# Attention and two gated products on one core: at a block border of the second product, VectorE does the border's sums first and the next operand's low halves after them

## The chip, the cores and the metric

The kernel runs on one core of one Trainium2 chip. The metric is the device time of one execution in microseconds (us). Smaller is better. The core's engines work in parallel and meet at semaphores: TensorE (PE in the profile; PEld is its weight load), VectorE (DVE), ScalarE (ACT), GpSimd (POOL) and SyncE (SP), which here only issues DMAs.

## The reference

```python
def _moe_ref(x, w_in, w_out) -> np.ndarray:
    h = x @ w_in
    g = h * np.cos(h)
    return (g @ w_out).astype(np.float32)
def _moe2_ref(x, w1, w2, w3, w_out) -> np.ndarray:
    h = np.maximum(np.maximum(x @ w1, x @ w2), x @ w3)
    return (h @ w_out).astype(np.float32)
def reference(**kwargs):
    ...
    attn_out = _attn_ref(**attn_kwargs)
    x = np.ascontiguousarray(attn_out.transpose(0, 2, 1, 3)).reshape(B * S, H * D)
    x = _moe_ref(x=x, **moe_kwargs)
    return _moe2_ref(x=x, **moe2_kwargs)
```

The attention is a chunked one over 3072 tokens. The first layer has 512 inputs, 2048 hidden features and 512 outputs, the second 512, 768 (three times) and 512. All in float32. The "second product" of this document is `g @ w_out` of the first layer.

## The kernel before

The program runs through stages: attention together with the first product `x @ w_in` and the gate (to about 360 us), the second product (to about 594 us), then the second layer. Every float32 operand of a product is split into a high part (a cast by ScalarE to the type fp32r) and a low part (what is left, a subtraction by VectorE), and each product is three matmuls, high by high, high by low and low by high (`three`, L617 to L619).

The second product is done with the seven products of Winograd's form of a 2 by 2 block multiplication. The tokens stand in six **blocks** of 512 (`NBLK1`, index b). Each block has eight **units** (`FPAIRS`, index i, in all 48 units n = 8 b + i); a unit adds the contribution of 256 hidden features. In a unit TensorE does the products in the order 1, 6, 7, 5, 2, 3, 4 (`ORDER1`), each into a PSUM bank of its own that stays open for all eight units, with six matmuls of 256 columns: 42 matmuls in a unit. In the last unit of a block each product's last matmul raises `whole_done[p]` (for product 4 it is `unit_done`), and in the first unit of the next block a bank is opened again only when its contents have been read (`open_bank`): bank 1 after `y1_copied`, 6 after `u2_done`, 7 after `u3_done`, 5 after `y5_copied`, 2 after `y11_done`, 3 after `y12_done`, 4 after `y21_done`. This place is a **block border**. The borders stand at units 7, 15, 23, 31, 39 and 47; here they are called border 0 to border 5. "Border 0" is thus the end of unit 7 and the start of unit 8.

The operand g of a unit is made by a pipeline. SyncE loads it from DRAM into one of two raw buffers (`load_g`, L365), VectorE makes its sums (`sums_g(n)`: four instructions of 256 columns, L1191 to L1197), ScalarE the high part in two pieces (`high_g`, L914) and VectorE the low part in two pieces (`low_g(n, 0)` and `low_g(n, 1)`, L1207, 1024 and 768 columns), the second of which raises `g_ready`. TensorE starts unit n only with `g_ready` at n + 1. Three operand slots take turns. The raw buffer is free when the low part is made: `load_g(n + 2)` waits for `g_ready` of n, so a load follows the low halves of the unit two before it.

VectorE's list is written out by hand. In turn n it makes the sums and low halves of unit n + 2, two units ahead of TensorE. At a border it also makes the border's sums: `u2` (L1334, waits for `whole_done[6]`), `u3` (L1337, `whole_done[7]`), `y11` (L1343, `whole_done[2]`), two sums in `y12` (L1345 and L1348, the second after `whole_done[3]`), `y22` (L1350) and `y21` (L1353, after `unit_done`). SyncE stores the four results one turn later (`store_y`, L374): its list there is `load_g(n + 4)` for border unit n, the stores of the border, then the next load.

Of the kernel before, what the change touches and what calls it, by code (L numbers as in the profile page):

```python
# [36 lines left out]
FPAIRS = NF // 2  # L37
# [5 lines left out]
UNITS1 = NBLK1 * FPAIRS  # L43
# [35 lines left out]
def program(nc, qk_in, v_in, w1_in, w2_in, y_dram, out):  # L79
    ctx = ExitStack()  # L80
    with ctx:
# [43 lines left out]
        def operand(i):  # L125
            return slot(i).rearrange("p (h q c) -> p h q c", h=2, q=7)
# [183 lines left out]
        def y_total(b):  # L310
            return 16 * sum(Y_PIECES[b % 2:b + 1:2])
# [796 lines left out]
        def _(dve):  # L1108
# [75 lines left out]
            def low_w1(p):  # L1184
                dve.wait_ge(w1_high, p + 1)
                w = operand(p)
                dve.scalar_tensor_tensor(out=w[:, 1, :, :], in0=raw_w1(p), scalar=-2 * PI, in1=w[:, 0, :, :].bitcast(F32),
                                         op0=ALU.mult, op1=ALU.subtract).then_inc(w1_ready, 1)
# [10 lines left out]
            def sums_g(n):  # L1199
                dve.wait_ge(g_landed[n % 2], 16 * (n // 2) + 16)  # L1200
                sums_cols(graw[n % 2], g_sums, 4 * n)

            def low_g(n, part):
                dve.wait_ge(g_high, 2 * n + part + 1)
                q = slice(0, 4) if part == 0 else slice(4, 7)
                g = operand(9 + n % 3)
                low = dve.tensor_tensor(g[:, 1, q, :], graw[n % 2][:, q, :], g[:, 0, q, :].bitcast(F32), ALU.subtract)  # L1207
                if part:
                    low.then_inc(g_ready, 1)

            def low_w2(u):
                dve.wait_ge(w2_high, u + 1)
                w = operand(SLOT_A[u])
                raw = raw_d[W2_RING[u]]
                dve.tensor_tensor(w[:, 1, :, :], raw, w[:, 0, :, :].bitcast(F32), ALU.subtract).then_inc(w2_ready, 1)

            def y_sum(blk, i):
                dve.wait_ge(y_landed, 32 * blk + 32)
                if i:
                    dve.wait_ge(y_sums, 4 * blk + i)  # L1220
                b11, b12, b21, b22, e = [raw_y[:, q, :, :] for q in range(5)]
                if i == 2:
                    dve.wait_ge(y_ready, 7 * blk + 2)
                if i == 3:
                    dve.wait_ge(y_ready, 7 * blk + 4)
                o, in0, in1 = ((e, b12, b11), (b12, b22, b12), (e, b22, e), (e, b21, e))[i]
                dve.tensor_tensor(o, in0, in1, ALU.subtract).then_inc(y_sums, 1)  # L1227

            def y_low(blk, p):
                dve.wait_ge(y_high, 7 * blk + YORDER.index(p) + 1)  # L1230
                y = y_slot(p)
                dve.tensor_tensor(y[:, 1, :, :], source_y(p), y[:, 0, :, :].bitcast(F32), ALU.subtract).then_inc(y_ready, 1)  # L1232
# [27 lines left out]
            for t in range(NBLK):  # L1260
                n = NSUB * (t + 1)
                last = t == NBLK - 1
                for f in range(NF):
# [11 lines left out]
                    if f % 2:  # L1275
                        i = FPAIRS * t + f // 2
# [44 lines left out]
            for n in range(UNITS1):  # L1321
                b, i = divmod(n, FPAIRS)
                if n == 0:
                    low_w1(6)
                elif n == 3:
                    low_w1(7)
                if n and n + 2 < UNITS1:
                    sums_g(n + 2)
                if i == FPAIRS - 1:
                    dve.wait_ge(whole_done[6], b + 1)  # L1330
                    dve.wait_ge(y1_copied, b + 1)
                    if b:
                        dve.wait_ge(y_stored[(b - 1) % 2], y_total(b - 1))
                    dve.tensor_tensor(y12, y11, ps[:, BANK1[6], :], ALU.add).then_inc(u2_done, 1)  # L1334
                    dve.wait_ge(whole_done[7], b + 1)
                    dve.wait_ge(u2_done, b + 1)
                    dve.tensor_tensor(y21, y12, ps[:, BANK1[7], :], ALU.add).then_inc(u3_done, 1)  # L1337
                if n and n + 2 < UNITS1:
                    low_g(n + 2, 0)
                    low_g(n + 2, 1)  # L1340
                if i == FPAIRS - 1:
                    dve.wait_ge(whole_done[2], b + 1)
                    dve.tensor_tensor(y11, y11, ps[:, BANK1[2], :], ALU.add).then_inc(y11_done, 1)  # L1343
                    dve.wait_ge(y5_copied, b + 1)
                    dve.tensor_tensor(y12, y12, p5_kept, ALU.add).then_inc(u25_done, 1)  # L1345
                    dve.wait_ge(whole_done[3], b + 1)
                    dve.wait_ge(u25_done, b + 1)
                    dve.tensor_tensor(y12, y12, ps[:, BANK1[3], :], ALU.add).then_inc(y12_done, 1)  # L1348
                    dve.wait_ge(u3_done, b + 1)
                    dve.tensor_tensor(y22, y21, p5_kept, ALU.add).then_inc(y22_done, 1)  # L1350
                    dve.wait_ge(unit_done, FPAIRS * (b + 1))
                    dve.wait_ge(y22_done, b + 1)
                    dve.tensor_tensor(y21, y21, ps[:, BANK1[4], :], ALU.add).then_inc(y21_done, 1)  # L1353
                if n == 17:
                    low_w2(0)
                if n in (30, 31):
                    y_sum(0, n - 30)
                elif n == 41:
                    y_low(0, 1)
                    y_low(0, 5)  # L1360
                elif n == 42:
                    y_sum(0, 2)
                    y_low(0, 2)
                    y_low(0, 6)
                elif n == 43:
                    y_sum(0, 3)
                    y_low(0, 3)
                    y_low(0, 7)
                elif n == 44:
                    y_low(0, 4)  # L1370
                elif n == 45:
                    low_w2(1)
                elif n == 47:
                    low_w2(2)
# [140 lines left out]
```

## Time and profile before

| | us |
|---|---|
| median of 3 runs | 953.59 |
| lowest and highest of them | 952.93, 955.41 |
| the profiled execution, its own time | 953.36 |
| its span, first to last instruction | 951.6 |
| TensorE busy in the span | 935.8 |
| VectorE busy | 681.8 |
| ScalarE busy | 512.8 |
| GpSimd busy | 183.5 |

The span is what the trace covers; 1.8 us lie around it. Busy times of engines overlap, so their sum is not the span. A start time in a row counts from the span's beginning.

### The profile page before, as it was taken

The numbers are of one execution on the slowest core, as the hardware profiler recorded it, in microseconds if no ns is written. First come the engines' busy times: TensorE is split into PE (matmuls) and PEld (weight loads), VectorE is DVE, ScalarE is ACT, GpSimd is POOL, SyncE is SP. The second block draws the span as 40 slices with busy tenths as digits, with TensorE's granted clock in tenths as the row PEclk, the third lists the DMA queues.
The fourth block names the chain that finished last, engine by engine and source line by source line (L and its number), as shares of the span: only waits on it lengthen the run. The fifth ranks groups of instructions, "written<-read, shape, count | busy, mean of one in ns | idle before, by whom it ended". The sixth has DMA issues, their size and how long they took to land.

```text
span 951.6 us, 21413 instructions
## 1 busy us (share of the span) xinstructions
PE 935.8 (98%) x9100; PEld 918.7 (97%) x9100; DVE 681.8 (72%) x938; ACT 512.8 (54%) x689; POOL 183.5 (19%) x207
## 2 busy tenths in 40 slices
PE   6999999999999999999999999999999999999998
PEld 5889999999999999999999999999999999999998
DVE  5767667676766789989988889767446347678771
ACT  3879697877868884434343345434224224444441
POOL 0011112121211212001100003931000002657720
PEclk8999999999999999999999999999999999999999
DMA  8953456454653443434364342331130201325522
GB/s 299 372 190 131 141 180 211 152 189 156 207 184 129 134 167 122 156 124 150 121 208 136 127 134 92 130 123 56 54 113 34 100 34 56 122 100 201 191 97 78
DMA packets 55422, 135.60 MB, mean 142 GB/s; under 512 B 5152, under 2 KB 14368, under 8 KB 55328
## 3 DMA queue, kind: packets, MB, share of 16 engines
q1 hardware_dynamic: 44960, 98.58, 30.6%
q0 software_dynamic: 10368, 35.66, 10.2%
q8 instruction: 72, 1.18, 0.5%
q14 instruction: 22, 0.18, 0.1%
HBM read 87.03 MB, written 47.19 MB: 141 GB/s over the span
## 4 chain that ended last, share of the span: by engine, by line
PE 80%; DVE 9%; ACT 5%; DMA 3%; issue 2%; SPq 0%; POOL 0%; DVEq 0%; ACTq 0%
PE ps L617 25%; PE ps L618 25%; PE ps L619 25%; DVE units L1207 3%; PE ps L658 2%; PE ps L631 2%; PE ps L669 1%; ACT units L914 1%; PE ps L644 1%; DMA out<-work 1%; DMA early_qk<-qk_in 1%; DVE units L1232 1%; DMA work<-w_in 1%; ACT work L894 1%; ACT work L889 1%
## 5 line engine op out<-in xcount | busy, mean ns | idle before, releaser
L617 PE MATMUL ps<-units 128*128 128x384 f32 (+1 forms) x1940 | 606.6, 313 | 4.3 <-DVE units L1159 1.4
L619 PE MATMUL ps<-units 128*128 128x384 f32 (+1 forms) x1940 | 601.3, 310 | 0.0
L618 PE MATMUL ps<-units 128*128 128x384 f32 (+1 forms) x1940 | 601.1, 310 | 0.0
L617 PEld LDWEIGHTS ps<-units 128*128 128x128 f32 x1940 | 368.0, 190 | 8.2 <-DVE units L1112 1.7
L618 PEld LDWEIGHTS ps<-units 128*128 128x128 f32 x1940 | 368.2, 190 | 0.0
L619 PEld LDWEIGHTS ps<-units 128*128 128x128 f32 x1940 | 368.0, 190 | 0.0
L914 ACT CAST units<-work 128x1024 fp32r<-128x1024 f32 x96 | 85.8, 939 | 119.6 <-DVE work L1193 107.2
L1063 ACT COPY work<-ps 128x384 f32<-128x384 f32 (+1 forms) x144 | 63.5, 454 | 147.4 <-PE ps L619 146.2
L1207 DVE TENSOR_TENSOR units<-work,units 128x1024 fp32r<-128x1024 f32 x96 | 102.1, 1104 | 9.4 <-ACT units L914 9.4
L514 POOL DMA_DIRECT2D g_dram<-work x64 | 46.7, 729 | 299.4 <-DVE work L1170 299.4
L1170 DVE SCALAR_TENSOR_TENSOR work<-work 128x768 f32<-128x768 f32 x64 | 61.2, 957 | 36.4 <-ACT work L896 36.4
L1165 DVE SCALAR_TENSOR_TENSOR work<-work 128x768 f32<-128x768 f32 x64 | 60.7, 949 | 35.2 <-ACT work L889 35.2
L886 ACT ACTIVATE work<-ps 128x768 f32<-128x768 f32 x64 | 51.7, 807 | 53.2 <-PE ps L619 53.2
L1386 DVE TENSOR_TENSOR work<-work,ps 128x384 f32<-128x384 f32 (+1 forms) x48 | 24.8, 517 | 57.3 <-PE ps L619 57.0
L889 ACT ACTIVATE work<-ps,rounder 128x768 f32<-128x768 f32 x64 | 57.3, 896 | 1.9 <-DVE work L1170 1.9
L896 ACT ACTIVATE work<-work 128x768 f32<-128x768 f32 x64 | 54.2, 846 | 2.0
L894 ACT ACTIVATE work<-work 128x768 f32<-128x768 f32 x64 | 54.6, 853 | 0.2
L538 POOL DMA_DIRECT2D work<-w_in x18 | 9.8, 547 | 221.2 <-DVE units L1232 130.5
L1242 DVE TENSOR_TENSOR units<-work,units 128x1792 fp32r<-128x1792 f32 x18 | 41.2, 2289 | 15.3 <-ACT units L954 15.3
L1407 DVE TENSOR_TENSOR work<-work,ps 128x384 f32<-128x384 f32 (+1 forms) x48 | 24.9, 518 | 26.4 <-PE ps L619 26.0
L1412 DVE TENSOR_TENSOR work<-work 128x1152 f32<-128x1152 f32 x24 | 34.8, 1452 | 0.8
L939 ACT CAST units<-work 128x768 fp32r<-128x768 f32 x28 | 22.9, 836 | 22.8 <-DVE work L1227 18.7
(88 smaller groups left out, 771.1 us busy)
## 6 DMA issues: line engine op xcount, KB each, us to landing
g_dram<-work POOLq DMA_DIRECT2D x64, 384.0 KB, 3.5
work<-g_dram SPq DMA_DIRECT2D x48, 512.0 KB, 3.8
work<-qk_in SPq DMA_DIRECT2D x18, 768.0 KB, 6.1
work<-w_in POOLq DMA_DIRECT2D x40, 256.0 KB, 3.6
h_dram<-work SPq DMA_DIRECT2D x24, 384.0 KB, 3.0
work<-h_dram SPq DMA_DIRECT2D x18, 512.0 KB, 4.4
work<-y_dram SPq DMA_DIRECT2D x8, 768.0 KB, 5.9
out<-work SPq DMA_DIRECT2D x24, 256.0 KB, 2.5
```

The source lines that it names most:

```text
L617: pe.matmul(o, wh, mh, start=start, stop=False, skip_group_check=onto)
L618: pe.matmul(o, wh, ml, start=False, stop=False, skip_group_check=onto)
L619: return pe.matmul(o, wl, mh, start=False, stop=stop, skip_group_check=onto)
L886: act.activation(hid(i), hidden_banks(i), ACT.Copy, scale=1.0 / (2 * PI)).then_inc(u_copied, 1)
L889: act.activation(ang(i), hidden_banks(i), ACT.Identity, scale=1.0 / (2 * PI), bias=rounder[:, :])\
L894: act.activation(ang(i), ang(i), ACT.Sin, scale=BELOW_PI).then_inc(sin_done, 1)
L896: act.activation(ang(i), ang(i), ACT.Square, scale=ROOT_TWO).then_inc(square_done, 1)
L914: act.copy(operand(9 + n % 3)[:, 0, q, :], graw[n % 2][:, q, :]).then_inc(g_high, 1)
L1063: act.copy(tile[:, 0:span_of(n)], bank).then_inc(copied, 1)
L1165: dve.scalar_tensor_tensor(out=ang(i), in0=ang(i), scalar=ROUND, in1=hid(i), op0=ALU.subtract, op1=ALU.subtract).then_inc(r_done, 1)
L1170: dve.scalar_tensor_tensor(out=hid(i), in0=ang(i), scalar=1.0, in1=hid(i), op0=ALU.subtract, op1=ALU.mult).then_inc(g_done, 1)
L1207: low = dve.tensor_tensor(g[:, 1, q, :], graw[n % 2][:, q, :], g[:, 0, q, :].bitcast(F32), ALU.subtract)
```

## The change

In the turn of a border unit, except the last border (unit 47, which has no unit n + 2), the two `low_g(n + 2, ...)` move from between `u3` and `y11` to behind `y21`. All else stays: the same instructions, waits and increments.

```diff
@@ -1335,7 +1335,7 @@
                     dve.wait_ge(u2_done, b + 1)
                     dve.tensor_tensor(y21, y12, ps[:, BANK1[7], :], ALU.add).then_inc(u3_done, 1)
-                if n and n + 2 < UNITS1:
+                if n and n + 2 < UNITS1 and not (i == FPAIRS - 1 and n + 2 < UNITS1):
                     low_g(n + 2, 0)
                     low_g(n + 2, 1)
                 if i == FPAIRS - 1:
@@ -1351,6 +1351,9 @@
                     dve.wait_ge(y22_done, b + 1)
                     dve.tensor_tensor(y21, y21, ps[:, BANK1[4], :], ALU.add).then_inc(y21_done, 1)
+                if i == FPAIRS - 1 and n + 2 < UNITS1:
+                    low_g(n + 2, 0)
+                    low_g(n + 2, 1)
                 if n == 17:
                     low_w2(0)
```

VectorE's list at border 0 before the change (L1334 is `u2`, L1337 `u3`, L1207 the two pieces of the low part, L1343 to L1353 the other sums, L1191 the first sum of the next operand):

```order
360 L1334 TENSOR_TENSOR work<-work,ps 128x512
361 L1337 TENSOR_TENSOR work<-work,ps 128x512
362 L1207 TENSOR_TENSOR units<-work,units 128x1024
363 L1207 TENSOR_TENSOR units<-work,units 128x768
364 L1343 TENSOR_TENSOR work<-work,ps 128x512
365 L1345 TENSOR_TENSOR work<-work 128x512
366 L1348 TENSOR_TENSOR work<-work,ps 128x512
367 L1350 TENSOR_TENSOR work<-work 128x512
368 L1353 TENSOR_TENSOR work<-work,ps 128x512
369 L1191 TENSOR_TENSOR work<-work 128x256
```

And with the change, at the same place:

```order
360 L1334 TENSOR_TENSOR work<-work,ps 128x512
361 L1337 TENSOR_TENSOR work<-work,ps 128x512
362 L1343 TENSOR_TENSOR work<-work,ps 128x512
363 L1345 TENSOR_TENSOR work<-work 128x512
364 L1348 TENSOR_TENSOR work<-work,ps 128x512
365 L1350 TENSOR_TENSOR work<-work 128x512
366 L1353 TENSOR_TENSOR work<-work,ps 128x512
367 L1207 TENSOR_TENSOR units<-work,units 128x1024
368 L1207 TENSOR_TENSOR units<-work,units 128x768
369 L1191 TENSOR_TENSOR work<-work 128x256
```

Five sums stand ahead of the two pieces that followed `u3`. Borders 1, 2 and 4 read the same; at border 3 one more instruction (L1227) follows the block in both. The lists of the other engines are unchanged. This is SyncE's before and after, from the loads ahead of border 0 to those behind border 1 (L365 loads an operand g, L374 stores a border's results):

```order
45 L365 DMA work<-g_dram 128x2x512 x11
46 L374 DMA y_dram<-work 128x2x256
47 L374 DMA y_dram<-work 128x2x128 x4
48 L374 DMA y_dram<-work 128x2x256
49 L365 DMA work<-g_dram 128x2x512 x8
50 L374 DMA y_dram<-work 128x2x256 x4
```

The last load of row 45 is the one of unit 11. It waits for the low part that has moved, and the stores of border 0 stand behind it in the same list.

## Rows read from the trace of the kernel before

**Rows 1.** The page, part 1: busy us, share of the span, instructions.

```profile
PE 935.8 (98%) x9100; PEld 918.7 (97%) x9100; DVE 681.8 (72%) x938; ACT 512.8 (54%) x689; POOL 183.5 (19%) x207
```

**Rows 2.** Timeline, TensorE, start and us: first matmuls of units 8, 9, 10.

```profile
390.24 0.28 PE L617 MATMUL ps<-units 128*128 128x256 f32 x1
...
397.02 0.28 PE L617 MATMUL ps<-units 128*128 128x256 f32 x1
...
402.06 0.28 PE L617 MATMUL ps<-units 128*128 128x256 f32 x1
```

**Rows 3.** Timeline, VectorE, around border 0.

```profile
389.30 0.68 DVE L1334 TENSOR_TENSOR work<-work,ps 128x512 f32<-128x512 f32 x1
390.08 0.69 DVE L1337 TENSOR_TENSOR work<-work,ps 128x512 f32<-128x512 f32 x1
390.68 2.09 DVE L1207 TENSOR_TENSOR units<-work,units 128x1024 fp32r<-128x1024 f32 x2
392.69 0.68 DVE L1343 TENSOR_TENSOR work<-work,ps 128x512 f32<-128x512 f32 x1
...
394.07 0.69 DVE L1348 TENSOR_TENSOR work<-work,ps 128x512 f32<-128x512 f32 x1
...
396.07 0.42 DVE L1191 TENSOR_TENSOR work<-work 128x256 f32<-128x256 f32 x1
```

**Rows 4.** Chain that ended last: start, us, what; from border 4 on.

```profile
549.86 0.70 DVE work L1334
...
581.77 2.10 DVE units L1207 x2
```

**Rows 5.** Timeline, VectorE, around border 4; idle before, and releaser.

```profile
549.86 0.69 DVE L1334 TENSOR_TENSOR work<-work,ps 128x512 f32<-128x512 f32 x1 [1.51 <-PE ps L619]
550.65 0.69 DVE L1337 TENSOR_TENSOR work<-work,ps 128x512 f32<-128x512 f32 x1
...
553.26 0.68 DVE L1343 TENSOR_TENSOR work<-work,ps 128x512 f32<-128x512 f32 x1
...
556.04 0.69 DVE L1353 TENSOR_TENSOR work<-work,ps 128x512 f32<-128x512 f32 x1
556.65 0.42 DVE L1191 TENSOR_TENSOR work<-work 128x256 f32<-128x256 f32 x1
...
560.65 0.42 DVE L1191 TENSOR_TENSOR work<-work 128x256 f32<-128x256 f32 x1
```

**Rows 6.** Timeline, TensorE: products 6 and 2 of unit 39, unit 46's start.

```profile
549.54 0.28 PE L619 MATMUL ps<-units 128*128 128x256 f32 x1
...
551.70 0.28 PE L619 MATMUL ps<-units 128*128 128x256 f32 x1
...
583.38 0.28 PE L619 MATMUL ps<-units 128*128 128x256 f32 x1
583.92 0.39 PE L617 MATMUL ps<-units 128*128 128x256 f32 x1 [0.26 <-DVE units L1207]
584.14 0.28 PE L618 MATMUL ps<-units 128*128 128x256 f32 x1
```

**Rows 7.** Timeline, SyncE: the load behind border 0's low part, first store.

```profile
392.86 0.36 SPq L365 DMA_DIRECT2D work<-g_dram  x1
393.39 0.36 SPq L374 DMA_DIRECT2D y_dram<-work  x1
```

**Rows 8.** Line L365, landing times: border 0's load, border 4's, all of 380 to 600.

```profile
DMA to landing us min/median/max: 4.3/4.3/4.3
DMA to landing us min/median/max: 4.0/4.0/4.0
DMA to landing us min/median/max: 3.6/3.8/5.6
```

**Rows 9.** Timeline, VectorE and TensorE, behind border 1 and at unit 21.

```profile
435.69 0.42 DVE L1191 TENSOR_TENSOR work<-work 128x256 f32<-128x256 f32 x1
...
437.35 0.28 PE L617 MATMUL ps<-units 128*128 128x256 f32 x1
...
452.20 3.18 DVE L1207 TENSOR_TENSOR units<-work,units 128x1024 fp32r<-128x1024 f32 x2
...
457.50 0.28 PE L617 MATMUL ps<-units 128*128 128x256 f32 x1
```

## The prediction, on record before the changed kernel ran

> **What bounds the kernel now.** I read the page first: TensorE is busy for 935.8 of 951.6 us [rows 1]. A change that adds and removes no instruction can only win or lose in TensorE's few stalls, so I looked for those of the second product. I took TensorE's timeline through the whole stage and marked each start that is more than 0.135 us behind the one before it (the normal distance is 0.12 us). There are two places, and only two.
>
> The first is border 0. Unit 8 starts at 390.24, unit 9 at 397.02, unit 10 at 402.06 [rows 2]. An undisturbed unit takes 402.06 - 397.02 = 5.04 us (42 matmuls by 0.12), unit 8 took 6.78, so 1.74 us are lost, where banks 2, 3 and 4 are opened again. The reader sees why in VectorE's timeline [rows 3]: it comes late to this border (u2 at 389.30 although product 6 had ended at 390.24 - 3.44 = 386.80), puts 2 us of low halves in, and then the sums that free the banks.
>
> The second is unit 46. TensorE would have gone on at 583.38 + 0.12 = 583.50, started at 583.92, and the next matmul came 0.22 later in place of 0.12 [rows 6]: 0.52 us lost. The chain of waits shows what it waited for: from u2 at border 4 (549.86) the chain runs through VectorE, and through casts of ScalarE between VectorE's own sums and lows, up to the low halves that end at 581.77 + 2.10 = 583.87 [rows 4]. In those 34 us TensorE is not on the chain. u2 itself started 0.04 us after product 6 had ended (549.54 + 0.28 = 549.82), after 1.51 us of idling [rows 5, 6]. So from border 4 to unit 46 **VectorE is the bound**, and its starting gun is TensorE's product 6 of unit 39.
>
> **Border 0 with the change.** VectorE has work in hand all the time, so its sums close up. u3 starts at 390.08 as before; an instruction that depends on nothing just made follows 0.60 later, one that does 0.79 (390.08 to 390.68, 389.30 to 390.08 [rows 3]). y11 starts at 390.68 and ends at 391.36. The second y12 sum starts 394.07 - 392.69 = 1.38 after y11, at 392.06, and ends at 392.75. y21 starts 556.04 - 553.26 = 2.78 after y11 [rows 5], at 393.46, and ends at 394.15. All three are in time: unit 8, undisturbed, opens banks 2, 3 and 4 at 390.24 + 2.88 = 393.12, 393.84 and 394.56. The three stalls go.
>
> What is late next are the low halves of unit 9. They start 0.61 after y21 (556.04 to 556.65), at 394.07, and end 2.09 later at 396.16, while TensorE is at unit 9 at 395.28. It waits, starts at 396.21 (0.05 after the end, as at unit 46) and pays the 0.10 of a restart. Unit 10 then starts at 396.21 + 0.10 + 5.04 = 401.35 in place of 402.06: **0.7 us gained**, and not 1.74. VectorE goes on with the next sums at 396.07 as before.
>
> **Borders 1 to 4 with the change.** Here VectorE is ahead and idles before u2. y11 now stands right behind u3, could start at 550.65 + 0.60 = 551.25, but its product 2 ends only at 551.70 + 0.28 = 551.98 [rows 6], so it starts at 552.02. That idle time used to be filled with low halves. y21 starts 2.78 later at 554.80, the low halves at 555.41, and the next sums 2.01 behind (390.68 to 392.69 [rows 3]), at 557.42 in place of 556.65 [rows 5]: VectorE leaves the border 0.77 us later, measured from TensorE.
>
> At borders 1, 2 and 3 cover hides this. At border 1 the low halves of unit 17 end at 435.69 + 0.77 + 0.08 = 436.54 and the unit starts at 437.35, 0.8 to spare. The tightest later place that I found is unit 21, with low halves that end at 452.20 + 3.18 = 455.38 against a start at 457.50 [rows 9]: 2.1 to spare, 1.35 with the delay. VectorE's round is 560.65 - 556.65 = 4.0 us against TensorE's 5.04, so it catches up 1 us in each unit. Without this cover the delay would cost 0.77 at each border.
>
> At border 4 there is no cover: the extra y sums and low parts of the next stage keep VectorE on the chain to unit 46, where TensorE already waits. **0.77 us lost.**
>
> **The load behind the moved halves.** At border 4 the load of unit 43 waits for the low halves of unit 41. These now end at 555.41 + 2.09 = 557.50, the load starts 0.09 later (392.77 to 392.86 [rows 3, 7]), at 557.59. VectorE wants its data at 560.65 + 0.77 = 561.42, so it has 3.8 us. The load took 4.0 at this border and 4.3 at border 0, with one store close behind; over the stage it took 3.6 at least, 3.8 in the middle, and 5.6 at most [rows 8]. With the change all stores of the border are ready and follow it at once, so I take the upper of the two border values, 4.3: it lands at 561.89 and VectorE waits **0.5 us**, again on the chain. The bounds are nothing (3.6 to 3.8) and 1.8 (5.6). At border 0 the same wait meets slack: the low halves of unit 11 would end at 396.25 + 4.3 + 4.1 = 404.7, with the unit at 406.4, and with 5.6 at 406.0.
>
> A rule of the skill bears on this. The Trainium skill, "DMA: Bandwidth & Descriptors", section "Queues, rings and completion order", says that each DMA engine takes the descriptors of one issuing queue in ring order. By it the stores, all behind the load, would hardly slow it, and the sum would have 0 to 0.1 in this term, not 0.5. The trace only half agrees, as the border 0 load took 4.3 with a store 0.53 behind it.
>
> **The sum.** Unit 46 starts at 583.92 - 0.70 (border 0, which moves TensorE and with it border 4) + 0.77 + 0.50 = 584.49: **+0.6 us**. Everything behind it follows: unit 47 and the border's last sums hang on the same VectorE list, which is as late as TensorE is. Against the profiled execution this is 953.36 + 0.6 = 954.0. The median of the runs shown is 0.23 above that execution, so I give 954.2. 0.3% is 2.9 us, which is about what a measurement of this kernel can tell from no change (its three runs span 2.5 us).
>
> **The rivals.**
> - *As above, the load takes 3.9 to 4.7 at border 4*: +0.2 to +0.9, centre 954.2. Chance 0.5.
> - *The load is hidden* (ring order holds, 3.6 to 3.8): -0.70 + 0.77 = +0.1, 953.7. For it: unburdened loads took 3.8. Against it: all border loads that I read took 4 or more. Chance 0.18.
> - *The order of the two stretches does not trade one for one and border 0's gain stays*: the 0.77 would have to vanish, by VectorE catching up between border 4 and unit 46. Price -0.7, 952.9; if the stall at unit 46 went too, -1.2. Against it: VectorE stands on the chain through the whole stretch. Chance 0.1. All 2.26 us of stalls gone is the most that the change could give, and even that is under 0.3%.
> - *The other side: the load is slowed by the stores behind it.* All four results are stored at once, and one load of the stage took 5.6 between other transfers. At 5.6 the wait at border 4 is 1.8, +1.9 in all, 955.5. The same at border 1 brings unit 21 to 455.38 + 0.77 + 1.8 = 457.95 against 457.50, another 0.5 with its restart: 956.0. It decides from a load of 3.8 us on, and passes 0.3% only from a load of about 5.9 (a wait of 2.0 at border 4 and of 0.8 with its restart at unit 21). Chance 0.2, of which 0.04 beyond 0.3%.
> - The move could also do nothing at border 0 if VectorE came there in time in other executions. Then 0.7 is missing: +1.3, 954.9. Chance 0.02, as it is late by 2.5 us.
>
> **How the numbers follow.** Predicted 954.2. The likely case and the first two rivals lie from 952.9 to 954.5, the late load up to 956.0; with the scatter of the runs I give 952.8 to 955.9. Faster by over 0.3%: 0.02 (no case reaches it). Slower by over 0.3%: 0.05. The rest, 0.93, is no change.
>
> **What the changed profile would show.** Right: no stall at banks 2 to 4 of unit 8, one of about 0.9 before unit 9; y11 idle by about 0.7 at borders 1, 3 and 4 with product 2 as its releaser; the load of unit 43 issued near 556.9; VectorE waiting for it; a stall before unit 46 of about 1.7 us, or part of it at unit 45. Wrong: a load that lands before VectorE asks, stalls at units 17, 21, 33 or 41, or a stall in unit 8 that stays. What would make the prediction wrong is a change of an unseen kind, such as GpSimd's sums now meeting VectorE's at other times: at 452.20 two low pieces took 3.18 in place of 2.09 [rows 9].

## The result, and the profile after

The changed kernel is slower, by about 0.3%: median 956.62 us of 11 runs (954.74 to 958.16) against 954.15 of 11 runs of the kernel before (952.93 to 955.50), ratio 1.0027 with a 95% interval from 1.0018 to 1.0035. The forecast of 954.2 (952.8 to 955.9) was right in sign and too small: +0.6 us forecast, +2.5 measured. The measured median lies 0.7 us above the range.

The page of the changed kernel, part 1 (as [rows 1]) and two lines of part 4, the chain that ended last:

```profile
PE 938.0 (98%) x9100; PEld 920.8 (96%) x9100; DVE 682.0 (71%) x938; ACT 513.2 (54%) x689; POOL 187.5 (20%) x207
...
PE 75%; DVE 12%; ACT 5%; DMA 4%; issue 2%; SPq 1%; POOL 0%; DVEq 0%; ACTq 0%
PE ps L617 23%; PE ps L619 23%; PE ps L618 23%; DVE units L1207 5%; DMA work<-g_dram 3%; ACT units L914 2%; PE ps L658 2%; PE ps L631 2%; PE ps L669 1%; PE ps L644 1%; DVE work L1193 1%; DVE work L1191 1%; DMA early_qk<-qk_in 1%; DMA work<-w_in 1%; ACT work L894 1%
```

VectorE has the same work, but more of the chain runs over it (12% against 9%), and a new link stands in it: the loads of the operand g (`work<-g_dram`), 3% of the span, none of which the page of before listed.

TensorE's timeline shows where it stood still. Each row is the first matmul after a stall, in brackets the idle time and its releaser:

```profile
397.85 0.39 PE L617 MATMUL ps<-units 128*128 128x256 f32 x1 [0.65 <-DVE units L1207]
...
518.67 0.38 PE L617 MATMUL ps<-units 128*128 128x256 f32 x1 [0.26 <-DVE work L1353]
...
520.68 0.39 PE L617 MATMUL ps<-units 128*128 128x256 f32 x1 [1.03 <-DVE units L1207]
...
587.96 0.39 PE L617 MATMUL ps<-units 128*128 128x256 f32 x1 [1.31 <-DVE units L1207]
```

They answer to [rows 2, 6]. The three stalls in unit 8 have become one before unit 9 (397.85), and the one before unit 46 has grown (587.96), with a small one (0.21 us) now at 581.35 ahead of it. The two in between are new: they stand at **border 3**, one at bank 4 of unit 32 and one before unit 33. Nothing stood there before.

A stall costs more than its idle time, since the row in brackets counts only from the end of the last matmul, and a restart adds 0.1. So in this document the cost of a stall is counted from start to start: each distance of two matmuls over 0.135 us, less the normal 0.12. Summed by place, in the two profiles that are compared here:

| us lost by TensorE | before | changed | difference |
|---|---|---|---|
| border 0 (units 8, 9) | 1.75 | 0.91 | -0.84 |
| borders 1, 2 | 0 | 0 | 0 |
| border 3 (units 32, 33) | 0 | 1.89 | +1.89 |
| before units 45, 46 | 0.52 | 1.78 | +1.26 |
| sum | 2.27 | 4.58 | +2.31 |

The sum is of the size of the measured 2.5 us. The two profiled executions, 953.36 and 957.14 us, are 3.8 apart. Matched matmul by matmul, TensorE of the changed one was already 1.8 us later when it came to border 0 (this arose in the first 100 us, where nothing was changed). It was 0.9 later behind border 0, 2.8 behind border 3, 4.0 from unit 46 on, and between 4.0 and 4.1 from there to 900 us. So what the order costs lies in the second product alone.

Why border 3? VectorE's timeline of the changed kernel, from border 2 to border 3:

```profile
471.53 0.68 DVE L1334 TENSOR_TENSOR work<-work,ps 128x512 f32<-128x512 f32 x1
...
483.68 0.43 DVE L1191 TENSOR_TENSOR work<-work 128x256 f32<-128x256 f32 x1 [1.28 <-DMA work<-g_dram]
...
488.06 0.43 DVE L1191 TENSOR_TENSOR work<-work 128x256 f32<-128x256 f32 x1 [0.28 <-DMA work<-g_dram]
...
499.15 0.43 DVE L1191 TENSOR_TENSOR work<-work 128x256 f32<-128x256 f32 x1 [2.98 <-DMA work<-g_dram]
...
513.76 0.68 DVE L1334 TENSOR_TENSOR work<-work,ps 128x512 f32<-128x512 f32 x1
...
517.93 0.69 DVE L1353 TENSOR_TENSOR work<-work,ps 128x512 f32<-128x512 f32 x1
518.53 2.09 DVE L1207 TENSOR_TENSOR units<-work,units 128x1024 fp32r<-128x1024 f32 x2
```

And TensorE's, the last matmul of product 6 at each of these two borders, which u2 (L1334) waits for:

```profile
469.83 0.28 PE L619 MATMUL ps<-units 128*128 128x256 f32 x1
...
510.15 0.28 PE L619 MATMUL ps<-units 128*128 128x256 f32 x1
```

VectorE's timeline of the kernel before, at the same two borders:

```profile
468.67 0.42 DVE L1197 TENSOR_TENSOR work<-work 128x256 f32<-128x256 f32 x1
469.23 0.69 DVE L1334 TENSOR_TENSOR work<-work,ps 128x512 f32<-128x512 f32 x1
...
509.55 0.69 DVE L1334 TENSOR_TENSOR work<-work,ps 128x512 f32<-128x512 f32 x1 [0.67 <-PE ps L619]
```

There u2 started 0.04 us after product 6 had ended, at both borders. VectorE had idled 0.13 us before it at border 2 (468.67 + 0.42 = 469.09 to 469.23) and 0.67 at border 3.

In the changed kernel product 6 ended at 470.11 at border 2 and u2 started at 471.53, 1.4 us late. At border 3 it ended at 510.43 and u2 started at 513.76, **3.3 us late**. In between VectorE waited three times for a load of g, 4.5 us in all; before, it waited once there, 1.7 us, for the load of unit 30. The three loads belong to units 27, 28 and 30. SyncE's line L365 gives their times from issue to landing: unit 27's 5.2, unit 28's 3.9, unit 30's 6.9, against a middle value of 3.8 [rows 8].

```profile
DMA to landing us min/median/max: 5.2/5.2/5.2
DMA to landing us min/median/max: 3.9/3.9/3.9
DMA to landing us min/median/max: 6.9/6.9/6.9
```

The middle one was quick but issued late. SyncE's timeline shows why: six stores stand between the load of unit 27 (478.48) and that of unit 28 (484.18), and issuing them took until 484.

```profile
478.48 0.36 SPq L365 DMA_DIRECT2D work<-g_dram  x1
478.89 5.18 SPq L374 DMA_DIRECT2D y_dram<-work  x6
484.18 0.44 SPq L365 DMA_DIRECT2D work<-g_dram  x1
```

The load of unit 30 stands behind the two loads of y (768 KB each), in both kernels. Before, it took 5.6 us [rows 8]. It took 6.3 to 6.9 in the three profiles in which border 2 was moved and SyncE's list left as it is, and 5.4 to 6.0 in the eight in which border 2 was not moved. Why it takes longer there stays open.

One more party shows in the trace. The DMA engines also carry packets of 16 KB of the instruction queue (q8 on the page), one in about every 15 us. This is the count for 479.39 to 481.5 in the changed kernel (packets, MB, share):

```profile
q8 instruction: 1, 0.02, 6.1%
```

That packet lasted from 479.39 to 481.46. It lies over the load of unit 27, and over a store instruction of SyncE that took 2.4 us to issue from 479.40 on. So the 5.2 us of this load may not be the stores' doing alone; e5 below bears on it.

### The profile page after: what moved, and what is told of

It is laid out like the page before. It is cut to its first block, busy times and chain, and to the rows that moved or that the text cites. A ratio compares the mean times of both kernels' runs of the same rounds, so it can differ in the third digit from the quotient of the medians.

```text
span 955.3 us, 21413 instructions
## 1 busy us (share of the span) xinstructions
PE 938.0 (98%) x9100; PEld 920.8 (96%) x9100; DVE 682.0 (71%) x938; ACT 513.2 (54%) x689; POOL 187.5 (20%) x207
## 4 chain that ended last, share of the span: by engine, by line
PE 75%; DVE 12%; ACT 5%; DMA 4%; issue 2%; SPq 1%; POOL 0%; DVEq 0%; ACTq 0%
PE ps L617 23%; PE ps L619 23%; PE ps L618 23%; DVE units L1207 5%; DMA work<-g_dram 3%; ACT units L914 2%; PE ps L658 2%; PE ps L631 2%; PE ps L669 1%; PE ps L644 1%; DVE work L1193 1%; DVE work L1191 1%; DMA early_qk<-qk_in 1%; DMA work<-w_in 1%; ACT work L894 1%
## 5 line engine op out<-in xcount | busy, mean ns | idle before, releaser
L1207 DVE TENSOR_TENSOR units<-work,units 128x1024 fp32r<-128x1024 f32 x96 | 102.1, 1104 | 7.5 <-ACT units L914 7.5
```

## The experiments

Theory A: the lateness of VectorE is carried from border to border, through the 0.8 us that it leaves each border later and through the loads that are issued later and meet the stores and the y loads. Theory B: border 3 stalls by its own move. Theory C: the 2.5 us do not come from the second product. Twelve more runs were made (e1 to e4, e5 to e8 and e9 to e12 together), each group beside the kernel before on one chip. In most, the condition of the moved low halves names the units at which they move (here e1's):

```diff
-                if n and n + 2 < UNITS1 and not (i == FPAIRS - 1 and n + 2 < UNITS1):
+                if n and n + 2 < UNITS1 and n not in (7,):
...
-                if i == FPAIRS - 1 and n + 2 < UNITS1:
+                if n in (7,):
```

The results in one table: the ratio to the kernel before with its interval, and TensorE's losses by place in the one profile of each kernel, counted as above.

| kernel | moved at borders | ratio (95%) | border 0 | border 2 | border 3 | units 45 to 47 |
|---|---|---|---|---|---|---|
| before | none | | 1.75 | 0 | 0 | 0.52 |
| changed | 0 to 4 | 1.0027 (1.0018 to 1.0035) | 0.91 | 0 | 1.89 | 1.78 |
| e1 | 0 | 0.9998 (0.9989 to 1.0006) | 1.53 | 0 | 0 | 0.53 |
| e2 | 3 | 1.0004 (0.9994 to 1.0015) | 2.01 | 0 | 0 | 0.53 |
| e3 | 4 | 1.0018 (1.0009 to 1.0027) | 2.15 | 0 | 0 | 1.79 |
| e4 | 1, 2 | 1.0040 (1.0026 to 1.0054) | 2.8 | 0.88 | 2.08 | 0.52 |
| e5 | 0 to 4, stores late | 1.0012 (1.0003 to 1.0021) | 1.06 | 0 | 1.04 | 1.28 |
| e6 | 0 to 4, y loads apart | 1.0008 (1.0000 to 1.0017) | 1.16 | 0.25 | 0.07 | 1.87 |
| e7 | 0 to 4, both edits | 1.0011 (1.0002 to 1.0019) | 0.97 | 0 | 1.15 | 1.29 |
| e8 | 0, 3, 4 | 1.0001 (0.9992 to 1.0010) | 1.41 | 0 | 0 | 1.91 |
| e9 | 0 to 4, again | 1.0027 (1.0016 to 1.0037) | 1.80 | 0.57 | 0.95 | 1.92 |
| e10 | 0, 1, 3, 4 | 1.0015 (1.0006 to 1.0024) | 1.39 | 1.26 | 0 | 1.87 |
| e11 | none, y low later | 1.0003 (0.9994 to 1.0012) | 1.65 | 0 | 0 | 0.36 |
| e12 | 0, y low later | 0.9983 (0.9974 to 0.9992) | 1.24 | 0 | 0 | 0.34 |

Border 0 in e4 includes 0.3 us of small gaps at the first products of unit 8. Left out in e9 are 0.3 us at 379.94, before the border.

The profile is one execution, the ratio a comparison of many. For all thirteen rows below the first the stall sum of the profile, less that of before, comes within 1 us of the timed difference; the worst are e8 (+1.05 against +0.1), e12 (-0.7 against -1.6) and e10 (+2.25 against +1.4).

**e1, border 0 alone.**

> The low halves stand behind the border's sums at border 0 alone; the other borders are as before the change. Theory A (lateness of VectorE is carried from border to border: the move at a border delays the low halves, these the next loads, and VectorE reaches border 3 too late): border 0 alone wins, since only there VectorE was late before. Its stalls fall from 1.74 us to about 0.9, none appears at border 3, the stall at unit 46 stays at 0.5: 0.8 us faster, about 0.9992 of the kernel before. Theory B (the new stalls at border 3 belong to that border's own move): the same here. Theory C (the 2.5 us do not come from the second product at all): this kernel is slower too, by some part of 2.5 us.

953.18 us against 953.42: no difference that is clear of noise. As theories A and B both had it, border 3 and unit 46 are as before. The gain at border 0 is small in this profile (1.53 against 1.75), because VectorE came to it later: u2 started 3.0 us after product 6 had ended, against 2.5 before. The columns of the table show that this place scatters: with the old order it cost 1.65 to 2.8 us in five profiles of kernels that are alike up to there (before, e2, e3, e4, e11), and 0.9 to 1.8 in the nine with the new order. The means are 2.07 and 1.27, so the gain is 0.8 in the profiles; the timed runs of e1 (-0.2 us, from -1.0 to +0.6) neither show nor exclude it. Theory C falls: this kernel is not slower, and the matmul-by-matmul comparison above finds the rest of the program unchanged.

**e2, border 3 alone** (`n in (31,)`).

> The low halves are moved at border 3 alone. Theory A: VectorE comes to border 3 in time (it idled 0.67 us there before), leaves it 0.8 us later, unit 33 has 0.8 us to spare: no stall there or one under 0.2 us; the stalls stay at 1.7 us in border 0 and 0.5 us at unit 46, and the time is that of the kernel before within 0.3 us. Theory B: the 1.8 us of stalls that the changed kernel shows at border 3 (0.5 at bank 4, 1.3 at unit 33) appear here too: 1.8 us slower, 1.0019.

953.99 against 953.42, and no stall at border 3. VectorE idled 0.65 us before u2 there, so it was in time. Theory B, which had 1.0019 and 1.8 us of stalls there, fails: the ratio is 1.0004, at most 1.0015.

**e3, border 4 alone** (`n in (39,)`).

> The low halves are moved at border 4 alone. Both theories: VectorE leaves border 4 0.8 us later and waits some 0.4 us for the load behind, and the stall at unit 46 grows from 0.5 to 1.6 to 1.8 us: 1.1 to 1.3 us slower, about 1.0012. If VectorE could catch up between border 4 and unit 46, the time would be that of before.

955.00 against 953.42, +1.6. VectorE's timeline, y11 at border 4 and the first sum of unit 43:

```profile
551.64 0.69 DVE L1343 TENSOR_TENSOR work<-work,ps 128x512 f32<-128x512 f32 x1 [0.68 <-PE ps L619]
...
561.52 0.43 DVE L1191 TENSOR_TENSOR work<-work 128x256 f32<-128x256 f32 x1 [0.41 <-DMA work<-g_dram]
```

The prediction has both terms: the idle time before y11 and the wait for the load (0.4 us here). Together they grow the loss before units 45 and 46 from 0.52 to 1.79, and it is not caught up.

**e4, borders 1 and 2** (`n in (15, 23)`).

> The low halves are moved at borders 1 and 2 and at no other. Theory A: VectorE waits about 0.5 us for the load behind border 1 and 1.3 us for that behind border 2, and waits 2 to 3 us for the load of unit 30 behind the two large loads of y; it reaches border 3 some 3 us later than before. With that border's old order the sums then come too late for banks 2 to 4, so stalls of 1 to 2 us stand at border 3 although nothing was moved there: 1.0010 to 1.0020. Theory B: nothing was moved at border 3, so there is no stall there, and the time is that of before within 0.3 us.

957.05 against 953.42. This is the strongest evidence: border 3 has its old order, and yet it stalls. Border 0 has its old order too, and u2 at border 2 is 2.3 us late, by border 1's move alone. TensorE's timeline in this kernel:

```profile
517.68 0.39 PE L617 MATMUL ps<-units 128*128 128x256 f32 x1 [0.47 <-DVE work L1343]
...
519.08 0.39 PE L617 MATMUL ps<-units 128*128 128x256 f32 x1 [0.42 <-DVE work L1348]
...
520.47 0.39 PE L617 MATMUL ps<-units 128*128 128x256 f32 x1 [0.42 <-DVE work L1353]
```

Banks 2, 3 and 4 are late one after the other, as at border 0 before the change. VectorE waited 2.5 us for unit 30's load and started u2 at 513.55 with no idle time. The size (1.0040) is beyond what I expected: it has 0.88 at border 2 as well, none of the gain at border 0, and the largest loss at border 0 of all profiles.

**e5, the stores later.**

```diff
-                if n % FPAIRS == 2 and n > 2:
+                if n % FPAIRS == 5 and n > 5:
                     store_y(n // FPAIRS - 1)
```

> The changed kernel with the stores of a border three turns later in SyncE's list, so that the loads of the next three units have no store behind or before them. Theory A says that part of VectorE's lateness comes from loads that share the DMA engines with four or six stores: the load behind each border falls from 4.2 to 5.2 us to about 3.8, the next one from 3.9 to 5.1 to 3.8, the waits for loads of 0.3 to 1.3 us behind borders 0, 1, 2 and 4 go, and VectorE comes 1.5 to 2 us earlier to border 3. The stalls there fall from 1.9 us to under 0.5, unit 46's by 0.4: 1.5 to 2.2 us faster than the changed kernel, 1.0003 to 1.0010 of the kernel before. The rival (the stores do not matter, the 0.8 us that VectorE leaves each border later is all): as the changed kernel, 1.0027.

954.64 against 953.39, 1.0012 where the changed kernel has 1.0027. The waits right behind borders 0, 1 and 4 are gone (two of 0.3 to 0.4 us stand a few units behind border 0 instead, where the stores now are) and unit 46's loss is 0.5 smaller, so the stores are part of it. But 1.04 stays at border 3 where I had expected under 0.5, because the waits for the loads of units 27 and 30 are still there:

```profile
480.53 0.43 DVE L1191 TENSOR_TENSOR work<-work 128x256 f32<-128x256 f32 x1 [0.94 <-DMA work<-g_dram]
...
495.97 0.43 DVE L1191 TENSOR_TENSOR work<-work 128x256 f32<-128x256 f32 x1 [3.34 <-DMA work<-g_dram]
```

The edit did not take the stores away from unit 30's load. It put the six of border 2 right behind it, as SyncE's timeline shows, and the load took 7.2 us:

```profile
488.72 0.37 SPq L365 DMA_DIRECT2D work<-g_dram  x1
489.14 4.41 SPq L374 DMA_DIRECT2D y_dram<-work  x6
```

The load of unit 27 took 4.8 us, although no store was near it. A packet of the instruction queue lay over it (477.05 to 478.32). The loads behind borders 0 and 1 took 3.71 and 3.75, against 4.25 and 4.37 in the changed kernel: this is what the stores add.

**e6, the two y loads two turns apart** (`load_y` gets the part as an argument).

```diff
-                if n == 3 * FPAIRS + 4:
-                    load_y(0)
+                if n == 3 * FPAIRS + 3:
+                    load_y(0, (0,))
+                elif n == 3 * FPAIRS + 5:
+                    load_y(0, (1,))
```

> The changed kernel with the two large loads of y (768 KB each), which stand one behind the other ahead of the load of unit 30, two turns apart. Theory A: the 3.0 us that VectorE waits for unit 30's operand become two waits that sum to about 1.5 us; it reaches border 3 about 1.5 us earlier, and the stalls there fall from 1.9 to about 0.5 us: 1.4 us faster than the changed kernel, about 1.0012 of the kernel before. If the y loads play no part, as the changed kernel, 1.0027.

954.60 against 953.39. Border 3's loss falls from 1.89 to 0.07. In place of 0.28 and 2.98 VectorE waits three times, 0.25, 0.31 and 0.72 (this kernel's L1193 is L1191 of the others):

```profile
486.09 0.42 DVE L1193 TENSOR_TENSOR work<-work 128x256 f32<-128x256 f32 x1 [0.25 <-DMA work<-g_dram]
...
490.49 0.43 DVE L1193 TENSOR_TENSOR work<-work 128x256 f32<-128x256 f32 x1 [0.31 <-DMA work<-g_dram]
...
495.30 0.43 DVE L1193 TENSOR_TENSOR work<-work 128x256 f32<-128x256 f32 x1 [0.72 <-DMA work<-g_dram]
```

So with the two y loads apart most of border 3's stall goes, in this profile and, as 1.0008 against 1.0027, in the timed runs. The lateness itself is only halved: u2 at border 3 started 1.5 us late, against 3.3.

**e7, both edits.**

> The changed kernel with both edits, stores three turns later and y loads apart. Theory A: no stall at border 3; what stays is border 0 (0.9 to 1.5 us of stalls, against 1.7 to 2 before) and unit 46 (1.3 us against 0.5): the time of the kernel before within 0.5 us, 0.9997 to 1.0005.

954.68 against 953.39, no better than either alone, which I had not expected. The stores of border 2, three turns later, now stand right ahead of the second y load, and the load behind these took 6.5 us in its profile: 1.15 at border 3. The two edits are not independent, since each only picks the turn in which a burst of transfers falls.

**e8, borders 0, 3 and 4** (`n in (7, 31, 39)`).

> The low halves are moved at borders 0, 3 and 4, and borders 1 and 2 keep their order. Theory A: VectorE comes to border 3 in time, so its own move costs nothing there, and the three moves add up from the single ones: -0.3 (border 0), 0 to 0.5 (border 3), +1.3 to 1.6 (border 4): 1.2 us slower, 1.0010 to 1.0017. The stall sum at border 3 is under 0.2 us. If border 3 stalls need no lateness from borders 1 and 2, 1.0030.

953.93 against 953.39, and nothing lost at border 3. VectorE's timeline there:

```profile
509.57 0.69 DVE L1334 TENSOR_TENSOR work<-work,ps 128x512 f32<-128x512 f32 x1 [0.67 <-PE ps L619]
510.36 0.69 DVE L1337 TENSOR_TENSOR work<-work,ps 128x512 f32<-128x512 f32 x1
511.73 0.69 DVE L1343 TENSOR_TENSOR work<-work,ps 128x512 f32<-128x512 f32 x1 [0.68 <-PE ps L619]
```

u2 starts when product 6 is done, with idle time to spare: exactly the picture that the prediction had drawn for all borders. Its profile has 1.05 us more stalls than before's, the timed runs give +0.1 with an interval from -0.8 to +1.0; my 1.2 us (1.0010 to 1.0017) lies at or above the end of that interval.

**e9, the changed kernel again.**

> The changed kernel once more, beside the next three, for a second profile of it. If the lateness is a property of the order and not of one execution, the profile shows the same chain: VectorE waits about 1 us for the load behind border 2 and 2.5 to 3.5 us for unit 30's, starts the sums of border 3 about 3 us late, and stalls of 1.3 to 2.2 us stand at border 3. Time 1.0020 to 1.0035 of the kernel before.

956.54 against 954.02, the same ratio of 1.0027. The chain is there again, u2 at border 3 being 2.4 us late, but the stalls are split otherwise: 0.57 at border 2 and 0.95 at border 3, less than the 1.3 that I had expected for border 3 alone. Which border shows the stall depends on the execution, their sum (1.5, and 1.9 in the first profile) much less.

**e10, all but border 2** (`n in (7, 15, 31, 39)`).

> The changed kernel with border 2 alone in its old order. Theory A in the form that the eighth run leaves (no stall at border 3 when neither border 1 nor 2 is moved): if border 2's move is what counts, because its low halves delay the loads of units 27 and 28 and these meet the two y loads, VectorE is in time at border 3, no stall there: as with borders 0, 3 and 4 moved, 1.0001 to 1.0010. If the lateness from border 1 alone carries that far, VectorE starts border 3's sums over 1.5 us late and 0.5 to 1.5 us of stalls stay: 1.0015 to 1.0025.

955.55 against 954.02. Neither form of the expectation was right. Border 3 is free of stalls, but 1.26 us are lost at **border 2**, whose order was not changed:

```profile
476.07 0.39 PE L617 MATMUL ps<-units 128*128 128x256 f32 x1 [0.33 <-DVE work L1348]
...
477.46 0.38 PE L617 MATMUL ps<-units 128*128 128x256 f32 x1 [0.41 <-DVE work L1353]
```

VectorE comes 2.0 us late to this border, where it had 0.13 us to spare before the change. Both moves ahead of it have a part: behind border 0 VectorE waited 2.2 us for three loads and came to border 1 with no time to spare. That border 1's move alone is enough is shown by e4, not by this run. Border 3 was in time although its own order was changed.

**e11, the other stall.** The low part of y for product 7 is made in turn 44, not 43, in the kernel before:

```diff
                     y_low(0, 3)
-                    y_low(0, 7)
                 elif n == 44:
+                    y_low(0, 7)
                     y_low(0, 4)
```

> The kernel before with one low part of y (product 7's, 0.95 us of VectorE) made a turn later, behind the low halves of unit 46 in place of ahead of them. If VectorE's list is what holds unit 46 back, these low halves end 0.87 us earlier and the stall of 0.5 us there goes: 0.5 us faster, 0.9995. If something else sets unit 46, no change.

953.81 against 954.02, ratio 1.0003: no difference. The stall at unit 46 is gone, so VectorE's list did hold it, but 0.36 came back at unit 47.

**e12, border 0 and e11's edit.**

> The low halves moved at border 0 alone, and the y part a turn later: the two gains that the runs point to. Border 0 gives 0.3 to 0.8 us, unit 46 gives 0.5: 0.8 to 1.3 us faster, 0.9987 to 0.9992 of the kernel before. If VectorE's list behind unit 46 is as tight as ahead of it, the 0.5 us come back as a stall at unit 47 or at the start of the next stage, and 0.3 us at most are left.

952.38 against 954.02, ratio 0.9983 (0.9974 to 0.9992): faster than both kernels. Its profile has one large stall left, before unit 9:

```profile
395.39 0.38 PE L617 MATMUL ps<-units 128*128 128x256 f32 x1 [0.99 <-DVE units L1207]
```

The stall sum of 1.58 explains 0.7 of the 1.6 us. The rest is within the interval (0.8 to 2.5 us), and no run shows a cause for it. The profile cannot give one: this execution was already 1.0 us ahead of the profiled one of before when it came to border 0, which is scatter from execution to execution.

## Why the prediction was right or wrong

**What bounds the kernel** held: all of the difference that the change makes is in stalls of TensorE behind VectorE.

**Border 0** held. The three stalls went, one before unit 9 came, at 0.91 in this profile and 1.27 in the mean of nine, against 2.07 in the mean of five with the old order. 0.7 was predicted and 0.8 found, though the place scatters by as much (e9, in the new order, lost 1.80).

**Border 4** held. y11 idled 0.68, as computed, and the next sums started 7.56 us after u2 in place of 6.79: the 0.77. The load behind took 4.3 as taken, and VectorE waited 0.39 for it (0.5 predicted). The loss there grew by 1.26, against the computed 1.27. That the two agree to 0.01 is luck: the wait was 0.1 shorter, and a second stall, at 581.35, added a restart of 0.1.

**The step that failed** is "At borders 1, 2 and 3 cover hides this", with its ground that VectorE "catches up 1 us in each unit". I checked the cover of each border against TensorE's needs just behind it (units 17 and 21) and not against VectorE's arrival at the *next* border. The idle time before u2 is what is left of the cover after a block, and it was 1.54 us at border 1 but only 0.13 at border 2 and 0.67 at border 3. The gain of 1 us in each unit was there, 8.3 us in a block (8 units by 5.04 us against 8 by 4.0), but from border 1 to border 2 it was spent: 4.8 us on the border's own sums, 1.9 on a low part of w2, 1.9 on sums and low halves that took longer while GpSimd made sums of its own (from 450.55 on). The lateness adds up. From border 1: 0.77 plus waits for loads of 0.47 and 0.22, less the 0.13, gives 1.3, and u2 at border 2 was 1.4 late. From border 2: 1.4 plus 1.28 + 0.28 + 2.98 - 1.67 of additional load waits, less the 0.67, gives 3.6; u2 at border 3 was 3.3 late. With an arrival so late, the new order loses at border 3 what the old one lost at border 0. e4 and e10 show the lateness travelling to a border that was not changed, e2 and e8 that border 3 stands its own move when VectorE is in time. Of the signs that the prediction named for being wrong, a stall at unit 33 came true.

**The load term** was too small for that reason too. I charged one load, at border 4, and put those behind borders 1 to 3 at nothing, within the same cover. What the move takes from a load is its lead. At border 4 the load was issued 7.2 us before VectorE asked for its data; with the change it was 3.9, about as long as a load takes. The load itself changed little: the first behind each border took 4.31, 4.24, 4.19, 4.32 and 3.96 us before, with a store or two close behind, and 4.25, 4.37, 5.18, 4.18 and 4.29 with all stores behind it. There is a second load for each border (issued when the stores allow it): 5.1, 4.7, 3.9, 4.9 and 4.7 us to landing, against 3.7 to 3.9 before. And the load behind the y loads took 6.9 in place of 5.6. Each of the edits e5 and e6 takes away a part of this: by the ratios 1.4 and 1.8 us of the 2.5 go, by the medians 1.2 and 1.3.

**The rivals.** "The load is slowed by the stores" named one of the right agents with the wrong place. Its worst case of 956.0 had the stall at unit 21, which did not come. "The load is hidden" fell: the load with the stores behind it took 4.2 to 5.2 us at all five borders. The Trainium skill, "DMA: Bandwidth & Descriptors", section "Queues, rings and completion order", states that each DMA engine takes the descriptors of a ring in order. No run here shows the order in which the pieces start. The runs do show that it does not spare a load the transfers issued behind it: 4.25 and 4.37 us with the stores behind (borders 0 and 1), 3.71 and 3.75 with the stores moved away (e5).

TensorE's clock played no part: the granted clock was 1.00, the upper of its two levels, in every stretch of 25 us from 375 to 594 us in both profiled executions (0.996 and 0.994 over the whole program), the stalls of up to 1.3 us included.

## What to carry to other kernels

When an edit makes an engine later that is not the bound, its slack must be followed to the next place where that engine is waited for *with all that lies between*: the idle time ahead of the next meeting point, not the slack right behind the edit, is the budget, and it must cover the delays of all earlier meeting points together. An operand's last consumer also sets when its buffer is loaded again, so each moved release must be charged with the transfers that it now collides with. A rule that wins where an engine comes late (border 0) loses where it comes early (border 4), and should be applied only where the trace shows which of the two holds.

## What the runs showed that was not expected

A load of 512 KB issued ahead of four or six stores of the same queue was slowed by them, from 3.8 to between 4.2 and 4.4 us at four borders; one or two stores close behind had already done as much before the change. At border 2, where it took 5.2, a packet of the instruction queue lay over it as well. Loads under such a packet are slower even where nothing else runs beside them. In the fourteen profiles 353 loads of g issued from 392 us on had no other transfer under way beside them. A packet counts as over a load when it meets it for 0.3 us or more, later than 1 us after the issue. Of the 283 loads without one, two took more than 4.0 us (4.1 and 4.3). Of the 70 loads with one, 24 did, up to 5.2. This is a coincidence in time, counted and not tested by an edit.

One of SyncE's store instructions at border 2 took 2.4 us to issue, against 0.4 to 0.5 for most, which held back the next load by 1.8 us (issued at 484.18; the low halves that it waits for ended at 482.40). All nine stores of the fourteen profiles around the borders that took 1.3 us or more to issue met a packet of the instruction queue. And border 0, which is the same in five kernels, lost between 1.65 and 2.8 us from one profiled execution to the next, a spread of about half the effect under study.
